# Two weight loads moved to later rounds of the attention, and the inverses fetched with one transfer instead of two

## The reference

```python
scores = scale * q @ k.T + bias        # bias: slope of the head times the distance
scores = where(is_global | is_local, scores, -1e9)    # first 8 positions, and the last 96
a = exp(scores - max); a = a / (sum(a) + 1e-9)
x = (a @ v) -> [tokens, heads * 64]
x = silu(x @ w_in1) @ w_out1
x = (h * clip(h + 3, 0, 6) / 6) @ w_out2,  h = x @ w_in2
```

## Time and profile before

| | us |
|---|---|
| median of 3 runs | 581.81 (581.61 to 583.2) |
| the profiled execution | 582.91 |
| its span | 581.0 |
| TensorE busy | 572.3 |
| VectorE / ScalarE / GpSimd busy | 369.5 / 329.0 / 260.9 |

### The profile page before, as it was taken

The page is one execution under the profiler, slowest core; times in us unless marked ns, Lnnn a source line. Parts: engine busy times, 40 slices in busy tenths (PEclk is TensorE's granted clock), DMA queues, the critical chain, the costliest instruction groups (busy, mean ns, idle before and its releaser), DMA issues.

```text
span 581.0 us, 9616 instructions
## 1 busy us (share of the span) xinstructions
PE 572.3 (99%) x3438; PEld 517.9 (89%) x3438; DVE 369.5 (64%) x682; ACT 329.0 (57%) x639; POOL 260.9 (45%) x258
## 2 busy tenths in 40 slices
PE   8979999999999999999999999999999999999998
PEld 6758899999999999999999999999998999999996
DVE  7868898667544867576555686575459675555331
ACT  7858876454444665444555666454556664555441
POOL 6546757669333036295333317494331344331110
PEclk9989999999999999999999999999999999999999
DMA  6778421422221013213212203212111243111002
GB/s 237 251 293 266 148 101 67 144 73 74 73 73 64 28 55 110 72 38 96 59 64 74 72 9 138 72 44 87 54 70 37 74 157 132 56 55 37 1 2 108
DMA packets 16995, 53.25 MB, mean 92 GB/s; under 512 B 2130, under 2 KB 2738, under 8 KB 16946
## 3 DMA queue, kind: packets, MB, share of 16 engines
q1 hardware_dynamic: 16514, 51.83, 26.6%
q10 hardware_dynamic: 432, 0.79, 0.4%
HBM read 49.41 MB, written 3.19 MB: 91 GB/s over the span
## 4 chain that ended last, share of the span: by engine, by line
PE 93%; DMA 3%; ACT 1%; DVE 1%; SPq 1%; issue 0%; POOL 0%; DVEq 0%; POOLq 0%
PE ps L1177 40%; PE ps L1268 23%; PE ps L1259 15%; PE ps L1260 8%; PE ps L1149 2%; DMA inv_rows<-turned 2%; PE ps L1127 2%; PE ps L1103 2%; ACT probs L875 1%; DMA inverses<-inv_rows 1%; SPq L290 0%; DVE negs L642 0%; PE ps L1135 0%; SPq L231 0%; DMA words<-in_counts 0%
## 5 line engine op out<-in xcount | busy, mean ns | idle before, releaser
L428 POOL TENSOR_TENSOR wo_lo<-wo_raw,wo_hi 128x1024 fp32r<-128x1024 f32 x32 | 76.8, 2399 | 237.2 <-ACT wo_hi L935 237.2
L1177 PE MATMUL ps<-x_hi,wi_hi 128*128 128x384 f32 x448 | 150.3, 335 | 0.0
L1177 PE MATMUL ps<-x_lo,wi_hi 128*128 128x384 f32 x448 | 149.9, 335 | 0.0
L1177 PE MATMUL ps<-x_hi,wi_lo 128*128 128x384 f32 x448 | 149.8, 334 | 0.0
L618 DVE TENSOR_TENSOR c_sb<-ps,p_c 128x384 f32<-128x384 f32 x64 | 35.7, 557 | 151.5 <-PE ps L1177 151.4
L915 ACT ACTIVATE p_c<-ps 128x384 f32<-128x384 f32 x64 | 31.5, 492 | 121.5 <-PE ps L1177 121.5
L1177 PEld LDWEIGHTS ps<-x_hi,wi_hi 128*128 128x128 f32 x448 | 84.1, 188 | 1.7 <-issue 0.3
L1177 PEld LDWEIGHTS ps<-x_hi,wi_lo 128*128 128x128 f32 x448 | 84.1, 188 | 0.5
L1177 PEld LDWEIGHTS ps<-x_lo,wi_hi 128*128 128x128 f32 x448 | 84.1, 188 | 0.0
L1020 ACT ACTIVATE g_hi<-g_f 128x768 fp32r<-128x768 f32 x64 | 50.6, 839 | 46.3 <-DVE g_f L628 25.9
L1268 PE MATMUL ps<-wo_hi,g_lo 128*128 128x512 f32 (+1 forms) x194 | 75.3, 388 | 0.0
(11 more groups left out here) (112 smaller groups left out, 1043.3 us busy)
## 6 DMA issues: line engine op xcount, KB each, us to landing
wi_raw<-in_w_in SPq DMA_DIRECT2D x32, 512.0 KB, 3.4
wo_raw<-in_w_out SPq DMA_DIRECT2D x32, 512.0 KB, 3.3
v_raw<-in_v SPq DMA_DIRECT2D x8, 704.0 KB, 4.9
k_raw<-in_kT SPq DMA_DIRECT2D x7, 464.0 KB, 5.0
inverses<-inv_rows SPq DMA_DIRECT2D x24, 128.0 KB, 3.0
out_y<-y_out SPq DMA_DIRECT2D x11, 256.0 KB, 5.3
q_raw<-in_qT SPq DMA_DIRECT2D x6, 384.0 KB, 5.9
q_raw<-in_qT ACTq DMA_DIRECT2D x1, 384.0 KB, 4.6
```

Source lines behind the costliest of these rows:

```text
L428: nc.gpsimd.tensor_tensor(wo_lo[:, s % 2, :], wo_raw[:, s % 2, :], wo_hi[:, s % 2, :], ALU.subtract).then_inc(wo_lo_ok, 1)
L1177: mm = nc.tensor.matmul(p_bank(bank), w[:, s % 2, at], x[:, b, k, :], start=fresh and k == 0 and i == 0, stop=k == 1 and i == 2, skip_grou ...
```

## The change

On SyncE, the load of the first W_out moves from behind m = 1 to behind m = 3, and that of the second to behind m = 6; the second W_in stays behind m = 1. They are written in two tables now. ScalarE's `wo_high(0)` moves from pass 5 to pass 6. `rows_in` issues one transfer instead of two: its source is both heads' rows with a repeat of 64 between, its target all 128 partitions of `inverses`, and the scaling waits for 16 instead of 32 on the semaphore. The instructions of the other engines stay as they are (line numbers of the changed kernel are higher by 1 to 3).

```diff
--- before.py
+++ after.py
@@ -40,8 +40,11 @@
 X_WORK = {16: (("s", 0, 0), ("s", 0, 1)), 17: (("h", 0, 0), ("s", 1, 0)), 18: (("h", 1, 0), ("s", 1, 1)), 19: (("l", 0, 0),),
           20: (("l", 1, 0),), 21: (("h", 2, 0), ("h", 3, 0)), 22: (("l", 2, 0),)}
 
+
 QK_AT = {0: 3, 2: 4, 3: 5, 5: 6, 6: 7}
 V_AT = {1: 2, 2: 3, 4: 4, 5: 5, 7: 6, 8: 7}
+WI_AT = {1: (1,)}
+WO_AT = {3: (0,), 6: (1,)}
 
 
 
@@ -286,9 +289,7 @@
                 def rows_in(m):
                     sp.wait_ge(inv_out, 16 * (m + 1))
                     at_least(sp, x_ok, m - 1)
-                    for h in range(2):
-                        sp.dma_start(inverses[D * h:D * h + D, m % 2, :],
-                                     inv_rows[m, h].partition_broadcast(D)).then_inc(inv_in[m % 2], 16)
+                    sp.dma_start(inverses[:, m % 2, :], inv_rows[m].unsqueeze(1).broadcast_to([2, D, 4 * P])).then_inc(inv_in[m % 2], 16)
 
                 next_qk(2)
                 next_v(1)
@@ -299,10 +300,10 @@
                     rows_in(m)
                     if m in V_AT:
                         next_v(V_AT[m])
-                    if m == 1:
-                        load_wi(sp, 1)
-                        load_wo(sp, 0)
-                        load_wo(sp, 1)
+                    for s in WI_AT.get(m, ()):
+                        load_wi(sp, s)
+                    for s in WO_AT.get(m, ()):
+                        load_wo(sp, s)
 
             def general():
                 load_v(sp, 0)
@@ -664,7 +665,7 @@
             def x_scaled(m):
 
                 dve.wait_ge(pv_done, 2 * m + 2)
-                dve.wait_ge(inv_in[m % 2], 32 * (m // 2 + 1))
+                dve.wait_ge(inv_in[m % 2], 16 * (m // 2 + 1))
                 nc.vector.tensor_tensor(x_four(m), o_bank(m), inverses[:, m % 2, :], ALU.mult).then_inc(x_ok, 1)
 
             def banded():
@@ -962,7 +963,7 @@
                     exps(4 * m + 2)
                     copy_t(4 * m - 2)
                     exps(4 * m + 3)
-                    if m == 5:
+                    if m == 6:
                         wo_high(0)
                 x_high(0, B22)
                 keep(0, p1_c, 0, P1)
```

## The result

| | before | after |
|---|---|---|
| median, us | 581.71 (4 runs) | 624.87 (624.0 to 626.42, 4 runs) |
| ratio | | 1.074 (95% interval 1.071 to 1.077) |
| span of the profiled execution | 581.0 | 624.5 |
| TensorE busy | 572.3 | 585.9 |
| packets under 512 B | 2130 | 1770 |

The change makes the kernel 7.4% slower, 43 us. The forecast was 614.3, with 598 to 632: right in its direction and its cause, and 10.6 us short.

A forecast was written before the change was run, and what follows sets the result against it. TensorE, busy 7 to 9 tenths, bounds the kernel; two-engine transfers would pace attention's rounds. Their 103.9 us sum delays the end by 31, plus 1.5 slow clock: 581.8 + 32.5 = 614.3 us, range 598 to 632.

The forecast's parts named there:

- The number of engines: Merged inverses transfer: its source pattern begins with count 2, so 2 DMA engines carry it; 1770 small packets; chance 0.80.
- The sum of the rounds: Attention part: twelve transfers, eleven gaps and the loads on the two engines total 103.9 us, last data ending at 124.5.
- the transfer of 5.6 us: Each merged inverses transfer: 64 packets on each of two engines at 88 ns take 5.6 us.
- the gap of 1.7: Between inverses transfers: 0.5 us for the small store to land plus 1.2 for the next start.
- I add one stretch of slow clock behind the last wait: End of the attention part: TensorE at 0.52 of full speed for 3.3 us, costing 1.5 us.
- Both agree: Attention's end: last turning of inverses +31.0, last scaling done at 125.7 against down projection at 95.16, +30.5.
- rivals 1 and 3: Merged transfer: rival 1, 16 or 8 engines, 576.2 us, chance 0.11; rival 3, 4 engines, 581, chance 0.03.
- a round without v 4.5 and hidden, one with v 6.4: Four-engine rounds: 2.8 us transfer; rounds with v exceed 5.6 by 0.8, six cost 4.8.
- The W_outs' 5.6 us: Moving both W_outs from m = 1: three rounds take 16.8 us instead of 22.4, giving 576.2 alone.
- The hole would close: TensorE's hole near 35 us: 1 MB less ahead of the m = 2 store outweighs the copy's 3.54 us wait.

The follow-up runs named there:

- tail2: Changed kernel with VectorE's scalings of m = 10 and 11 both moved behind step 1's sums and step 0's low parts: 622.47 us, ratio 1.068.
- the doses: Changed kernel with two 64-partition transfers, the repeat of 64 written as 8 × 8, 4 × 16 or 2 × 32: 588.36, 604.89 and 639.82 us.
- outer4: Changed kernel with two 64-partition transfers, the repeat of 64 written as 4 × 16 (four DMA engines): 604.89 us.
- tail: Changed kernel with VectorE's first three sums of step 1 and step 0's low parts ahead of the scaling of m = 11: 623.59 us, ratio 1.070.

## Why the prediction was right or wrong

**The number of engines was right.** 1770 small packets, and 1794, 1842, 1938 for the three other counts: each one is what the outermost count of the pattern says. The Trainium skill (DMA: Bandwidth & Descriptors, "Why a DMA increments its semaphore by 16 and not by 1") states that the number of engines is the largest up to 16 that divides the slowest dimension of both patterns; the counts of these runs agree with it for 2, 4, 8 and 16. The advice of the same page ("Rules for kernel authors") to put one 128-partition transfer in the place of two halves fails here (1.074), where the source begins with 2, and on sixteen engines it is neither gain nor loss (0.9988).

**The sum of the rounds was right to 4%, in part by luck.** The fetches are 101.9 us apart from the first to the last, where the sum had 103.9 − 5.6 = 98.3. Rounds without any load took 7.01 and 7.02 (forecast 7.3): the transfer of 5.6 us measured 5.2, the gap of 1.7 measured 1.8. The round with v, a W, k and q took 11.75 (11.2), those with v alone 9.62 and 9.72 (9.2). So two errors of opposite sign met: eleven rounds at 7.0 instead of 7.3 are 3.2 us less, and the rest, most of it what the loads add, was 6.8 us too small (a v adds 2.6 and not 1.9, a W about 2.0 and not 1.4).

**The end failed.** "I add one stretch of slow clock behind the last wait", 1.5 us, stood for what measured 8.4. I had let the down projection wait for the last scaling alone, and not asked what is queued behind a waiting scaling on VectorE; for SyncE's queue I had asked it. Of the 43.5 us at the down projection this step is 6.9, the rounds another 4.1 beyond the sum (35.1 against 31.0). Forecast 32.5 and these two make 43.5. The prediction had a warning before it: "Both agree" holds the end of the last scaling (125.7) against the begin of the down projection before (95.16), but in the kernel before the last scaling began 7.3 us ahead of that, at 87.71, and had waited for TensorE and not for a transfer:

```profile
87.71 0.69 DVE L668 TENSOR_TENSOR x_raw<-ps,inverses 128x512 f32<-128x512 f32 x1 [0.78 <-PE ps L1149]
```

Scaling against scaling, the sum's own 125.7 is +37.3 (125.7 against 88.40, its end), and the changed kernel's last scaling ends at 131.52, +43.1, nearly the +43.5 of the down projection. That the two paths agreed was luck. The part from the first down projection on did keep its length, as forecast (486.0 us before and now). It is not free of transfers, though, as the text on the profile before has it: there the DMA engines are busy 0.60 of the first 95 us and 0.21 of the rest, and a W_in that is issued behind the last fetch held step 2 in `tail2`.

**The prices of rivals 1 and 3 failed.** They never came to be tested by the change itself, but by the doses: 8 engines cost 4.8 us of span and not a gain, 4 engines 21.7 and not nothing. The failed step is "a round without v 4.5 and hidden, one with v 6.4": in `outer4` these measure 5.8 to 5.9 and 7.5 to 8.0. The transfer was priced as packets × 88 ns, 2.8 us, and the pair's packets lie over 4.0; the v adds more than 1.9. For the one transfer on two engines the packets had no such pauses (5.2 for the 5.6), and this error did not show in the forecast.

**The W_outs' 5.6 us failed.** "The hole would close" took one wait of one execution as the price of 1 MB ahead of the store. Moving the megabyte gave 1.0008, moving it out of the rounds 0.9985, and removing the wait at the copy 1.0016. The forecast did not suffer, as it had not subtracted the gain. Why the store takes 5.25 us in one execution and 7.2 in another stays open.

## What to carry to other kernels

Count the outermost dimension of both patterns before merging two transfers, and price a transfer on k engines by what is queued behind it on them, not by itself. If a small store and its answer go round once per tile in a shared queue, and the round is near the pace of the compute engines, most of what is added on their engines is paid (4.8 us for a sum of 7.7, 21.7 for 23.2), even if the bytes in all stay the same. Read the length of a transfer from its first packet to its last, not from its packets times the time of one. When a transfer gets late, read on every engine the list behind the instruction that waits for it: what stands there and needs nothing of it is late too.

## What the runs showed of the hardware

With two engines the rate was 51 GB/s, 81 ns for 2 KB on each, where one transfer had them alone; two transfers on the same two engines took 6.4 us for the same packets instead of 5.2. After 2.56 and 2.85 us in which TensorE stood still its granted clock was 0.50 for about 3 us, and after 3.82 us (`tail`) 0.50 and 0.53 for 6 us; after a hole of 2.19 us (before 123.53) it was not seen to fall. And the same kernel's runs spread over 6 us in 582, with single waits for a store that differ by 2 us, so what one trace shows for one such wait is not yet a cost. The window behind that hole, from 123.50 to 126.50 in the changed kernel, shows the full clock:

```profile
123.50:126.50 3.00, 2.96 (x38) 2.72 (x38) 2.40 (x5) 2.36 (x5) 0.00 (x0) 1.00 0.71 192
```
